# An attention block with two mixing layers on one core: tables and layer norm on other engines, filler products and another order of stages

## The reference

```
scores = (q @ k.T) / 8                      # attention, per head
rel  = i - j                                # query minus key position
keep = (j < n_global) | (0 <= rel < n_local)          # 8 and 96
dist = n_local where (global and not local) else |rel|
scores = where(keep, scores - slope[h] * dist, -1e9)
x = softmax(scores) @ v                     # heads side by side: 512 channels

xn = (x - mean) / sqrt(var + 1e-6) * g_ln   # layer norm
x  = x + relu(xn @ w_ch1) @ w_ch2           # 512 -> 2048 -> 512

theta = x @ w_theta                         # second mixing layer
y = w_tok_r @ (x * cos(theta)) + w_tok_i @ (x * sin(theta))
u = x + y
out = u + relu(u @ w_ch)
```

## Time and profile before

| | |
|---|---|
| runs | 584.79 us median of 3 (580.12 to 584.83) |
| profiled execution | 582.78 us, span 581.0 us, mean granted TensorE clock 0.982 |
| PE busy | 552.2 us, 95% of the span |
| DVE busy | 248.1 us, 43% |
| POOL busy | 217.9 us, 38% |
| ACT busy | 165.0 us, 28% |

### The profile page before, as it was taken

One profiled execution on the slowest core, in us unless ns is written; L12 is line 12 of the kernel. 1 busy time (PEld: TensorE's weight loads), 2 busy tenths in 40 slices (PEclk: granted clock), 3 DMA queues, 4 the chain that ended last, 5 costly groups with the idle time before them and its releaser, 6 DMA issues.

```text
span 581.0 us, 8733 instructions
## 1 busy us (share of the span) xinstructions
PE 552.2 (95%) x3446; PEld 495.5 (85%) x3446; DVE 248.1 (43%) x599; ACT 165.0 (28%) x423; POOL 217.9 (38%) x215
## 2 busy tenths in 40 slices
PE   6879979999899898899999999999999999999997
PEld 5768868778788787799999999988799999999997
DVE  4556544645464544222222222345676652305034
ACT  2534434343352542111111111153444441001010
POOL 8874430200300302149700150022389798262500
PEclk9779989999999999899999999999999999999999
DMA  6444214322222100004300020000012222331202
GB/s 203 146 149 155 85 38 132 111 57 64 62 64 61 42 1 1 1 0 146 124 22 1 0 82 2 0 1 0 2 54 55 55 81 82 109 108 56 81 15 95
DMA packets 24810, 36.96 MB, mean 64 GB/s; under 512 B 2240, under 2 KB 17600, under 8 KB 24768
## 3 DMA queue, kind: packets, MB, share of 16 engines
q1 hardware_dynamic: 24768, 36.38, 20.4%
HBM read 33.23 MB, written 3.15 MB: 63 GB/s over the span
## 4 chain that ended last, share of the span: by engine, by line
PE 86%; POOL 6%; DVE 5%; issue 1%; ACT 0%; DMA 0%; DVEq 0%; POOLq 0%; ACTq 0%
PE bank L1435 17%; PE bank L890 12%; PE bank L1092 11%; PE bank L1110 11%; PE bank L873 9%; PE bank L1305 6%; PE bank L1458 6%; PE bank L548 4%; POOL xn L804 4%; PE bank L518 3%; PE bank L533 3%; PE bank L821 1%; DVE stats L762 1%; PE bank L1441 1%; PE bank L558 1%
## 5 line engine op out<-in xcount | busy, mean ns | idle before, releaser
L873 PE MATMUL bank<-xnT,w1h 128*128 128x256 f32 x384 | 75.9, 296 | 0.5 <-DVE hTl L853 0.4
L1435 PE MATMUL bank<-ring_h,z_hi 128*128 128x384 f32 x192 | 65.8, 343 | 0.0
L873 PEld LDWEIGHTS bank<-xnT,w1h 128*128 128x128 f32 x384 | 60.5, 194 | 5.8 <-issue 4.0
L1092 PE MATMUL bank<-xnT,w1h 128*128 128x384 f32 x256 | 65.2, 335 | 0.0
L1435 PE MATMUL bank<-ring_h,z_lo 128*128 128x384 f32 x192 | 64.4, 335 | 0.0
L1435 PE MATMUL bank<-ring_l,z_hi 128*128 128x384 f32 x192 | 64.1, 334 | 0.0
L812 POOL TENSOR_TENSOR rstd<-rtmp,minus_half 128x2 f32<-128x2 f32 x6 | 4.3, 714 | 144.0 <-DVE rtmp L781 144.0
L1221 POOL TENSOR_TENSOR trig<-x,trig 128x512 f32<-128x512 f32 x24 | 32.8, 1388 | 67.9 <-ACT trig L1261 67.9
L497 ACT ACTIVATE sp_buf<-sp_buf,row_max 128x256 f32<-128x256 f32 (+1 forms) x96 | 46.3, 483 | 41.7 <-DVE row_max L446 41.7
L873 PE MATMUL bank<-xnT,w1l 128*128 128x256 f32 x192 | 54.9, 286 | 0.0
L1208 POOL TENSOR_TENSOR ring_l<-raw,ring_h 128x768 fp32r<-128x768 f32 x24 | 46.9, 1952 | 2.0
(11 more groups left out here) (127 smaller groups left out, 1168.1 us busy)
## 6 DMA issues: line engine op xcount, KB each, us to landing
raw<-wtokT SPq DMA_DIRECT2D x24, 384.0 KB, 3.3
raw<-w SPq DMA_DIRECT2D x8, 1024.0 KB, 5.9
v_sb<-vwin SPq DMA_DIRECT2D x16, 256.0 KB, 2.6
k_sb<-kcols SPq DMA_DIRECT2D x16, 200.0 KB, 3.2
q_sb<-qT SPq DMA_DIRECT2D x24, 128.0 KB, 2.9
outT<-out_sb SPq DMA_DIRECT2D x16, 192.0 KB, 1.9
v_sb<-vwin SPq DMA_DIRECT2D x8, 192.0 KB, 2.5
k_sb<-kcols SPq DMA_DIRECT2D x8, 136.0 KB, 2.9
```

The costliest lines, as they stand in the source:

```text
L873: last = nc.tensor.matmul(bank_of(n)[:, 0:AN], wt[q][:, d, f * P:(f + 1) * P], xnT[:, AT * c:AT * c + AT, low, d, :], start=(d == 0 and m ...
L1092: last = nc.tensor.matmul(h_bank[f % 2][:, 0:CN], wt[slot][:, d, fs], tokens(low, d), start=first, stop=(d == DC - 1 and wt is w1l))
L1435: last = nc.tensor.matmul(bank, zt[b][:, s, r, ds], wt[j % RING][:, r, :], start=(s == 0 and r == 0 and m == 0), stop=False)
```

## The change

- `dist1` and `dist0` are both built by DVE, from two tensors that it prepares (`ahead`: the relative position, plus FAR where it is negative; `far1`: FAR where it is at least n_local), by sums, maxima and minima. `first_distances_pool` is gone. DVE also makes `bias0` of heads 0 and 1, POOL the remaining 12 tables. The masks of block 0 wait for DVE's tables alone.
- The fillers start from a tile of zeros that DVE writes as its first instruction, and no longer from the identity that POOL builds. There are 70 filler calls in eleven places for 43 in eight.
- In the head, scores of blocks 3 and 4 and the attends stand at other places between transposes.
- SP loads q and k of block 4 ahead of the first weights.
- Newton (now three instructions) and scaling stand on DVE for all chunks. For chunk 0 they follow the first half of the masks of block 4, and POOL begins the split of load 1 only when `xn` is written. For the other chunks they stand two steps behind the statistics. POOL keeps only the root.
- Blocks 8 to 23 have other steps, and the statistics of chunks 2 to 5 stand at r = 11 for 13. Block 5's scores stand at step 2 for 1. For chunk 1 the first two parts of `xn` are transposed at r = 21 for 20.
- The second half of a block's masks stands at the start of the step behind its scores, and no longer at the end.

```diff
-WARM = (11, 6, 3, 2, 3, 2, 2, 14)
+WARM = (16, 4, 3, 3, 2, 4, 3, 4, 3, 3, 25)
...
-            where = (20, 20, 22, 22) if c == 0 else (19, 20, 20, 22)
+            where = (21, 21, 22, 22) if c == 0 else (19, 20, 20, 22)
...
-        SCORES_AT = {place_at(k, (-10, -4, 0, 8)): k for k in range(8, BLOCKS)}
-        TRANSPOSE_AT = {place_at(k, (-5, -1, 5, 11)): k for k in range(8, BLOCKS)}
-        ATTEND_AT = {place_at(k, (-4, 0, 8, 12)): k for k in range(8, BLOCKS)}
-        BACK_AT = {place_at(k, (-3, 1, 9, 13)): k for k in range(8, BLOCKS)}
-        SCORES_AT.update({1: 5, 5: 6, 9: 7})
+        SCORES_AT = {place_at(k, (-12, -7, -2, 4)): k for k in range(8, BLOCKS)}
+        TRANSPOSE_AT = {place_at(k, (-7, -3, 2, 8)): k for k in range(8, BLOCKS)}
+        ATTEND_AT = {place_at(k, (-5, -2, 4, 10)): k for k in range(8, BLOCKS)}
+        BACK_AT = {place_at(k, (-4, -1, 5, 11)): k for k in range(8, BLOCKS)}
+        SCORES_AT.update({2: 5, 5: 6, 9: 7})
         TRANSPOSE_AT.update({3: 4, 6: 5, 9: 6, 13: 7})
         ATTEND_AT.update({5: 4, 8: 5, 11: 6, 15: 7})
         BACK_AT.update({6: 4, 9: 5, 12: 6, 16: 7})
-        SECOND_EXPS_AT = {place_at(k, (-8, -3, 2, 9)): k for k in range(8, BLOCKS)}
-        SECOND_EXPS_AT.update({3: 5, 6: 6, 10: 7})
-        STATS_AT = {16: 1, **{place_at(k, (0, 0, 0, 13)): k // PAIRS for k in range(11, BLOCKS, PAIRS)}}
+        SECOND_EXPS_AT = {place_at(k, (-10, -5 if k == 9 else -6, -1, 6)): k for k in range(8, BLOCKS)}
+        SECOND_EXPS_AT.update({4: 5, 6: 6, 10: 7})
+        STATS_AT = {16: 1, **{place_at(k, (0, 0, 0, 11)): k // PAIRS for k in range(11, BLOCKS, PAIRS)}}
...
+            load_qk(4)
             load_raw(sp, 0)
             sp.dma_start(g_col[:, :], g_ln).then_inc(gain_loaded, 16)
-            load_qk(4)
...
+            nc.vector.memset(sp_buf[:, 0, 0, 0, 0:P], 0.0).then_inc(fill_ready, 1)
+            dve.wait_ge(iota_ready, 3)
+            ahead = sp_buf[:, 0, 1, 0, :]
+            step(nc.vector.tensor_scalar(ahead, iota_rel, 0.0, FAR, ALU.is_lt, ALU.mult))
+            step(nc.vector.tensor_tensor(ahead, ahead, iota_rel, ALU.add))
...
-            dve.wait_ge(iota_ready, 3)
...
+            dist, first = dist1[:, :], far0[:, 0:P]
+            nc.vector.tensor_scalar(far1[:, :], iota_rel, n_loc, FAR, ALU.is_ge, ALU.mult)
+            nc.vector.tensor_scalar(first, iota_col, n_glob, FAR, ALU.is_ge, ALU.mult)
             step(nc.vector.tensor_scalar(over_f[:, 0:1], n_glob, float(G_CAP), None, ALU.is_gt))
-            step(nc.vector.scalar_tensor_tensor(over_f[:, 1:2], n_loc, float(L_CAP), over_f[:, 0:1],
-                                                ALU.is_gt, ALU.max))
-            step(nc.vector.scalar_tensor_tensor(over[:, :], n_loc, 1.0, over_f[:, 1:2], ALU.is_lt, ALU.max))
+            nc.vector.scalar_tensor_tensor(over_f[:, 1:2], n_loc, float(L_CAP), over_f[:, 0:1],
+                                           ALU.is_gt, ALU.max)
+            step(nc.vector.tensor_tensor(dist, ahead, far1[:, :], ALU.add))
+            nc.vector.scalar_tensor_tensor(over[:, :], n_loc, 1.0, over_f[:, 1:2], ALU.is_lt, ALU.max)
+            nc.vector.tensor_scalar(dist[:, P - G_CAP:P], first[:, 0:G_CAP], n_loc, None, ALU.max)
+            step(nc.vector.scalar_tensor_tensor(dist0[:, 0:P], first, n_loc, dist[:, P:WIN], ALU.max, ALU.min))
             dve.sem_inc(over_ready, 1)
-            keep, t0 = sp_buf[:, 0, 0, 0, :], sp_buf[:, 0, 1, 0, :]
-            dist = dist1[:, :]
-            first = sp_buf[:, 1, 1, 0, 0:G_CAP]
-            nc.vector.tensor_scalar(first, iota_col[:, 0:G_CAP], n_glob, None, ALU.is_lt)
-            step(nc.vector.tensor_scalar(t0, iota_rel, 0.0, None, ALU.is_ge))
-            step(nc.vector.scalar_tensor_tensor(keep, iota_rel, n_loc, t0, ALU.is_lt, ALU.mult))
-            nc.vector.tensor_scalar(far1[:, :], keep, -1.0, -FAR, ALU.add, ALU.mult)
-            step(nc.vector.tensor_tensor(dist, iota_rel, keep, ALU.mult))
-            nc.vector.tensor_scalar(far1[:, P - G_CAP:P], first, -1.0, -FAR, ALU.add, ALU.mult)
-            step(nc.vector.tensor_scalar(dist[:, P - G_CAP:P], first, n_loc, None, ALU.mult))
-            step(nc.vector.tensor_tensor(dist, dist, far1[:, :], ALU.add))
             dve.sem_inc(dist_ready, 1)
             for h in range(2):
                 table(nc.vector, bias1, dist1[:, :], h, tables_ready)
+            for h in range(2):
+                table(nc.vector, bias0, dist0[:, 0:P], h, tables_ready)
...
-        def first_distances_pool(pool):
...
-            pool.wait_ge(mask_step, 3)
-            nc.gpsimd.tensor_scalar(glob, iota_col, n_glob, None, ALU.is_lt)
-            step(nc.gpsimd.tensor_scalar(near, iota_rel0, n_loc, None, ALU.is_lt))
-            step(nc.gpsimd.tensor_tensor(local, near, ahead, ALU.mult))
...
-                if k == 0 and u == 1:
-                    dve.wait_ge(tables_ready, 2)
+                if k == 0:
+                    dve.wait_ge(tables_ready, 4 - 2 * u)
                 elif k < PAIRS:
-                    dve.wait_ge(pool_tables, 2 + 4 * hp)
+                    dve.wait_ge(pool_tables, 4 * hp)
...
-                table(nc.gpsimd, bias0, dist0[:, 0:P], h, pool_tables)
...
-            pool.wait_ge(tables_ready, 2)
+            pool.wait_ge(tables_ready, 4)
             split_raw(pool, 0)
             norm_root(pool, 0)
-            norm_newton(pool, 0)
+            pool.wait_ge(norm.xn_ready, 1)
             split_raw(pool, 1)
             split_raw(pool, 2)
             split_raw(pool, 3)
             for c in range(1, EARLY):
                 norm_root(pool, c)
-                norm_newton(pool, c)
-                norm_scale(pool, nc.gpsimd, c)
...
-        def norm_newton(pool, c):
+        def norm_newton(dve, c):
 
             t0 = c * AT
             r, v, w = rstd[:, t0:t0 + AT], rtmp[:, 0, t0:t0 + AT], rtmp[:, 1, t0:t0 + AT]
-            pool.wait_ge(norm.root_ready, c + 1)
-            nc.gpsimd.tensor_tensor(w, r, r, ALU.mult).then_inc(norm.newton_step, 1)
-            pool.wait_ge(norm.newton_step, 4 * c + 1)
-            nc.gpsimd.tensor_tensor(v, w, v, ALU.mult).then_inc(norm.newton_step, 1)
-            pool.wait_ge(norm.newton_step, 4 * c + 2)
-            nc.gpsimd.tensor_scalar(v, v, -0.5, 1.5, ALU.mult, ALU.add).then_inc(norm.newton_step, 1)
-            pool.wait_ge(norm.newton_step, 4 * c + 3)
-            nc.gpsimd.tensor_tensor(r, v, r, ALU.mult).then_inc(norm.newton_step, 1)
-
-        def norm_scale(eng, ops, c):
+            dve.wait_ge(norm.root_ready, c + 1)
+            nc.vector.scalar_tensor_tensor(w, v, -0.5, r, ALU.mult, ALU.mult).then_inc(norm.newton_step, 1)
+            dve.wait_ge(norm.newton_step, 3 * c + 1)
+            nc.vector.tensor_tensor(v, w, r, ALU.mult).then_inc(norm.newton_step, 1)
+            dve.wait_ge(norm.newton_step, 3 * c + 2)
+            nc.vector.scalar_tensor_tensor(r, v, 1.5, r, ALU.add, ALU.mult).then_inc(norm.newton_step, 1)
+
+        def norm_scale(dve, c):
 
             t0 = c * AT
-            eng.wait_ge(norm.newton_step, 4 * c + 4)
+            dve.wait_ge(norm.newton_step, 3 * c + 3)
             if c >= 1:
-                eng.wait_ge(turn_mm, turn["xT", c - 1, DC - 1] + 1)
+                dve.wait_ge(turn_mm, turn["xT", c - 1, DC - 1] + 1)
             for u in range(AT):
-                last = ops.tensor_scalar(
+                last = nc.vector.tensor_scalar(
...
-        def keep_busy(n, bank=banks[7]):
+        def keep_busy(n, bank=banks[7], tile=ident[:, :]):
 
             for _ in range(n):
-                nc.tensor.matmul(bank[:, 0:P], ident[:, :], ident[:, :], start=True, stop=True)
+                nc.tensor.matmul(bank[:, 0:P], tile, tile, start=True, stop=True)
...
+            pe.wait_ge(fill_ready, 1)
+            keep_busy(WARM[0], tile=sp_buf[:, 0, 0, 0, 0:P])
             scores(pe, 0)
             general_tensor(pe)
             scores(pe, 1)
+            pe.wait_ge(ident_ready, 2)
             keep_busy(WARM[1])
+            scores(pe, 2)
             transpose_probs(pe, 0)
-            scores(pe, 2)
+            keep_busy(WARM[2])
             attend(pe, 0)
-            keep_busy(WARM[2])
+            scores(pe, 3)
+            keep_busy(WARM[3])
             transpose_probs(pe, 1)
             transpose_back(pe, 0)
-            keep_busy(WARM[3])
-            scores(pe, 3)
+            keep_busy(WARM[4])
             attend(pe, 1)
-            keep_busy(WARM[4])
+            keep_busy(WARM[5])
             transpose_probs(pe, 2)
             transpose_back(pe, 1)
-            keep_busy(WARM[5])
+            keep_busy(WARM[6])
+            attend(pe, 2)
+            keep_busy(WARM[7])
+            transpose_probs(pe, 3)
+            transpose_back(pe, 2)
             scores(pe, 4)
-            transpose_probs(pe, 3, (0,))
-            attend(pe, 2)
-            transpose_probs(pe, 3, (1,))
-            transpose_back(pe, 2)
+            keep_busy(WARM[8])
             attend(pe, 3)
```

(54 more changed lines are left out.)

## The result

The changed kernel takes 561.0 us (median of 4 runs, 560.55 to 561.46), the one before 584.05 beside it. The ratio is 0.962, with a 95% interval of 0.957 to 0.966: 3.8% faster. The forecast was 564, with a range of 556 to 574. The profiled execution took 560.55 us, its span 558.7, and its mean granted clock was 1.000 for 0.982.

What follows compares the result with a forecast made beforehand. PE, busy 95% of the span, was taken as the bound, with only idle time and slow clock to win. 7.3 + 2.6 + 5.9 + 5.1 - 1.6 = 19.3 us off 582.8 gave 563.5, stated as 564; range 556 to 574.

Steps and rivals of the forecast that it cites:

- The head: Start up to block 4's transposes: 4.6 us less before the first `xn` transpose, 3.1 from full clock, 7.3 in all.
- The boundaries: Between chunks: gains of 2.6 us at chunk 1, 5.9 at chunks 2 to 4, 5.1 at chunk 5, less 1.6.
- The scaling: Scaling of `xn` on DVE at the boundaries: priced at 1.65 us for two instructions, from rows of 0.83 and 1.47 each.
- Step order: Step r = 20 of chunks 1 to 4: less attention cover, charged 0.4 us each, -1.6, between 0 and -4.
- the note in the prediction that the time would be 2 us better by that rule: Chunks 1 and 5: with POOL idle, scaling falls below 0.83 us, up to 1 us gained at each.
- The mechanism at chunk 1: Step 20's output group: the bank release it needs is queued behind the scaling on DVE, a new 2.2 us wait.
- The two falls that I counted: PE's clock at half behind the 3.11 and 4.36 us waits for `xn`; gains of 1.65 and 1.7 us without them.
- B: Five boundaries: scaling takes 2.95 us on DVE and releases queue behind it; 570 us, or 574 with clock falls; chance 0.16.
- C: Head: 27 more filler calls, 6.3 us of PE work, become the bound and the head gives nothing; 571 us; chance 0.12.
- D: Head at half clock throughout, 24 us of work costing 21 more; 585 us, no change; chance 0.03.
- E: Each of 16 blocks in the steps: PE waits for late DVE; slower from 1.2 us each, 590 at 1.6; chance 0.05.

Runs made afterwards that it cites:

- experiment 5: Changed kernel without the 54 filler calls behind the first block: 558.9 us; with only 18 of them, before chunk 0's `xn` transposes: 559.4 us.
- experiment 6: Changed kernel with only 12 first and 18 last filler calls: 558.1 us; also with first weights loaded ahead of v 2 and q and k 4: 555.0 us.
- experiment 7: Changed kernel without POOL's wait for `xn` before the second split, so POOL splits while DVE scales chunk 0: 562.9 us.
- experiment 1: Changed kernel with Newton and scaling of chunks 1 to 5 back on POOL, new step order and head kept: 564.25 us.
- experiment 4: Fillers put into the five waits for `xn`: old steps and norm with the new head 575.5 us; the kernel before 579.9 us.
- experiments 3: Changed kernel with old step tables and norm on POOL as before, only the new head kept: 581.7 us, ratio 0.9965.
- experiment 2: Changed kernel with the old step order, keeping Newton and scaling on DVE and the new head: 567.7 us, ratio 0.975.

## Why the prediction was right

**The head** (7.3 forecast). 44.61 - 37.16 = 7.45, at both points within 0.2 us. It is partly luck: the first fillers ended 1.0 us earlier than taken (6.4 for 7.4), and PE lost that again in handoffs, so that the sum over fillers and products came out the same. PE was the bound as stated, and experiment 5 shows that this was a cost of the change. One statement was wrong: the first weights do not land before POOL's tables are through. POOL stood idle 4.36 us for them, until 18.02. It cost nothing while the fillers hid it, and was the next bound in experiment 6. The prediction also read only one of two slow stretches of the head. The kernel before was at half clock here too (stretch, length, PE busy, granted clock, then DMA share and GB/s):

```profile
13.50:20.40 6.90, 4.86 (x30) 0.51 0.45 141
```

Half of 4.86, 2.4 us, of the 4.6 us won ahead of the first `xn` transpose is this clock; it is in the sum only because the head after was added up at full rate. What the new tables, the earlier fillers and the new order each bring is not shown: no run takes these three apart.

**The boundaries** (2.6 + 5.9 + 5.1 - 1.6 = 12.0 forecast). The span fell by 22.3; less the head that is 14.9. The 2.9 us too little lie in two terms.
- The scaling. In the changed kernel it is

```profile
L768 DVE TENSOR_SCALAR xn<-x,mean_var,rstd x12: 539/544/546, 29.1 to 211.4; 128x512 f32<-128x512 f32 x12
```

  1.00 for two, where I took the lower of two rows from beside POOL's splits, 1.65. That is 0.65 of the 0.9 us less at chunk 1 and of the 1.0 at chunk 5; the rest is small prices ahead of it (at chunk 1 it started 6.8 us behind the back transpose, for 7.1). The Trainium skill ("SBUF — State Buffer", section "Who interferes with whom") had called for this: by it a DVE instruction that holds the port pair shared with GpSimd, or that has two SBUF inputs while GpSimd reads, blocks against it. The rows of experiment 7 agree, for the scaling and for the Newton steps (that the scaling holds the pair is inferred from its slowing alone); the note in the prediction that the time would be 2 us better by that rule was the better sum.
- Step order. I charged 0.4 at four places, 1.6 in all, and none of them shows a wait: those for `xnT` stand in chunk 0 (0.88) and at chunk 5 (0.24).

Together these are 3.5 us for 2.9, so 0.6 went the other way, and no run says where.

**The mechanism at chunk 1** was right in place and size and only partly in cause. "The release is queued behind the scaling on DVE" holds for 0.3 of the 1.32 us; the rest is the handling of the group just done (experiment 1).

**The clock.** The two falls that I counted, 1.7 each, were real in the profile of before, but the count of two was luck. Beside the experiments the kernel before ran 41 times: at a granted clock of 0.987 or 0.988 it took 580.3 to 580.9 us, at 0.982 582.0 to 583.2, at 0.976 to 0.979 584.3 to 585.2. Fillers in its waits (experiment 4) won 2.6 us against its median, and 0.6 against its executions at 0.988. Taken alone, the head would not have had my term: it brought 0.6 us by medians. The changed kernel's longest wait behind the first filler is 1.3 us, and its clock stays at 1.00. That this is why both terms came in full fits experiments 3 and 4, but the other half, the new boundaries with the old head, was not run. I had not asked whether the terms depend on each other.

**The rivals.** B (waits in another form) did not happen, and experiment 2 shows what would have made it: the same DVE work under the old steps. C (fillers as the bound) was half right: without most of them and with a shorter first block the time is 2.8 us less (558.1 for 560.9), of the 5.8 that experiments 5 and 6 found in all. D is out: the head ran at 1.00 with fillers, and without them up to the 4.19 us wait. The Trainium skill ("TensorE: Matmul & The Clock Gate", section "Part 4: PE-mode transpose") has it that transposes do not engage the full clock; in the profile without fillers transposes are nearly half of PE's work from 10 to 22 us (4.6 of 9.8 us busy) and the granted clock is 1.00 there. It had been raised by fillers, so the row shows that work with many transposes kept it, and no run here shows transposes letting it fall. E (every block waits) left no trace: no wait for probabilities is in the list.

## What to carry to other kernels

Two repairs of one wait do not add up, and neither may be enough alone: beside the new head, the new step order alone came within 3 us of the full change and the faster engine alone within 7. Behind a wait that is gone, look for the next queue. On an in-order engine ask what stands behind the instruction that you move in; here it was a bank release of 0.4 us that PE wanted. And size fillers by the wait that they cover (calls x 0.117 x 2 us against the idle time), put them only where the clock fell in a profile, and look afterwards for a data row that was ready before the filler ended.

## What the runs showed of the hardware

- The clock behind a wait of PE is not settled by the wait's length alone. Behind 2.35 us the granted clock stayed at 1.00 in one kernel and went to half for 3.4 us in another; behind 1.79 us likewise. Behind the waits of 4.36 us (before) and 4.19 us (no fillers) it fell in the profiles. With fillers in the waits it did not fall at the five boundaries, where it had fallen at each. Behind two waits of 0.8 to 0.9 us in chunk 0 it fell in the profiles of experiment 2 and of the fillers in the head-only kernel, and not in the head-only kernel itself, whose waits there are the same. And it differs between executions of one kernel (0.976 to 0.988 for the one before).
- A fall of 3.4 us takes 1.7 us from a PE that is busy throughout, as worked out from the half rate. Five falls removed brought 6.2 us and two brought 2.6. The kernel before took 2.0 us less by median at 0.988 than at 0.982, which is two falls' worth of clock.
- A DVE instruction on 128 x 2 values took 1.13 us for 0.16 beside a GpSimd instruction on SBUF of 1.27 us, and the two ended within 0.01 us of each other. In proportion small instructions pay most (7 times, for 2.2 times in the scaling).
- With the same first fillers the first scores started between 6.3 and 7.4 us. The profile gives a granted clock of 1.00 from the start, although the first matmuls took 0.22 us each for 0.12 later: in this stretch the 1.00 cannot be trusted.
